# Turning the scaled keys of items 8 and up on VectorE instead of TensorE

## The chip, the cores and the metric

The kernel runs on one core of a Trainium2 chip. Its time is the device time of one execution in microseconds. It has five engines that work side by side: TensorE (PE: products, weights loaded by PEld), VectorE (DVE), ScalarE (ACT), GpSimd (POOL) and SyncE (SP, which only starts transfers here).

## The reference

Gated linear attention and two layers of a fully connected network behind it, all in float32. Batch 4, 8 heads, 768 positions, 48 numbers per head:

```python
f = 1.0 / (1.0 + np.exp(-f_logit))
for t in range(S):
    state = f[:, :, t, :, None] * state + np.einsum('bhd,bhe->bhde', k[:, :, t], v[:, :, t])
    y[:, :, t] = np.einsum('bhd,bhde->bhe', q[:, :, t], state)
# x = y as 3072 tokens x 384
h = x @ w_in                                   # 384 -> 2048
g = np.where(h >= 1, h, np.where(h <= -1, 0.0, (h + 1) ** 2 / 4))
x = g @ w_out                                  # 2048 -> 384
h = x @ w_in2
P = a[0] + a[1] * h + a[2] * h**2 + a[3] * h**3
Q = 1.0 + abs(b[0]) * abs(h) + abs(b[1]) * h**2
out = (P / (Q + 1e-06)) @ w_out2
```

## The kernel before

The attention is cut into 24 items: six chunks of 128 positions, each for four pairs of heads (GROUPS = 4; ITEMS = 24). An item holds two heads of all four batches. Keys, queries and gates lie with the head's 48 numbers on the partitions (one head at 0, the other at 64) and 4 x 128 positions as columns.

For each item the running product of the gates is formed (`scan`, L846, VectorE), the keys are multiplied by its inverse growth (`scale_keys`, L511, GpSimd, into k_s) and the queries divided by it (`newton`, `scale_queries`, L862 to L873, VectorE). TensorE then makes the scores inside the chunk (`scores`, L1066), VectorE masks them (`mask`, L885), and TensorE makes the outputs, from the state that the chunk starts with (L1080) and from the masked scores (L1085). The state is carried on by `deltas` (L1096): a product of keys and values over the 128 positions. For this the keys must have positions on the partitions, so k_s is turned: four 128x128 transposes on TensorE (`transposes`, L1050, into the PSUM bank at_bank) and a copy to SBUF by ScalarE (`copy_keys`, L614, into k_nat). VectorE adds the product to the state (`states`, L899). The last chunk needs no new state: items 20 to 23 have neither transposes nor state products.

The first network layer pair runs in 96 tiles of 128 hidden units x 512 tokens. A tile n is nine products into PSUM (`spline_first`, L1126), then ScalarE's ReLU and square (L646, L649), VectorE's join (`spline_join`, L917), ScalarE's rounding into a high part (L656), VectorE's rest (`spline_lo`, L925), and nine products into the accumulators (`spline_second`, L1143). TensorE runs the second products two tiles behind the first (LAG1 = 2). The second pair of layers follows with the lines L1165 and L1187.

From item 4 on each item is worked off inside a window of four tiles, item i = 4 + n // 4, at fixed stages n % 4. Nothing schedules the work but the order of the code on each engine, with semaphores between engines. TensorE runs in stage 0 the first products of the tile, the transposes and the scores of item i, and the second products of an older tile; in stage 1 only the products of tiles; in stage 2 first products, outputs and state products, then second products; in stage 3 products of tiles. VectorE runs in stage 0 the join, the mask of item i, the rest and the scan of item i + 1; in stage 1 the join and the rest; in stage 2 join, rest and the query scaling of item i + 1; in stage 3 the rest of y and the state addition of item i, then join and rest. k_s has two buffers, k_nat one: the copy into it waits until the state products of the item before have read it (delta_ready), and GpSimd scales the keys of item i + 2 only when item i has been turned (kt_ready) and its scores made.

Of the kernel before, what the change touches and what calls it, by code (L numbers as in the profile page):

```python
# [11 lines left out]
P = 128  # L12
BATCH, HEADS, SEQ, DH = 4, 8, 768, 48
HS = 64
PAIRS = BATCH * HEADS // 2
CK = 128
NC = SEQ // CK
# [33 lines left out]
GROUPS = 4  # L51
# [59 lines left out]
def build(nc, qT, kT, fT, vT, fC, kC, qC, vC, w1, w2, a, b, outT):  # L111
# [3 lines left out]
    with ctx:  # L115
# [171 lines left out]
        def k_natural(i):  # L287
            return k_nat_head if i == HEAD - 1 else k_nat

        def values(i):  # L290

            if 2 <= i < HEAD:
                return v_head[i - 2], v_loaded[i], 16, -1
            turn = i // 2 - (i >= HEAD)
            return v_in[i % 2], v_loaded[i % 2], 16 * (turn + 1), i - HEAD if i < HEAD + 2 else i - 2
# [190 lines left out]
        def _(pool):  # L486
# [14 lines left out]
            def scale_keys(i):  # L501
                if i >= ITEMS:
                    return
                u = i % 2
                pool.wait_ge(k_loaded[u], 32 * (i // 2 + 1))
                pool.wait_ge(growth_ready, GROUPS * (i + 1))
                before = i - HEAD if i < HEAD + 2 else i - 2
                if before >= 0:
                    pool.wait_ge(scores_ready, before + 1)
                    pool.wait_ge(kt_ready, min(before + 1, ITEMS - GROUPS))  # L510
                nc.gpsimd.tensor_tensor(k_scaled(i)[:, :], k_in[u][:, :], growth[u][:, :], ALU.mult).then_inc(k_ready, 1)  # L511

            def split_w1(k):
# [68 lines left out]
        def _(act):  # L582
# [24 lines left out]

            def copy_keys(i):
                if i >= ITEMS - GROUPS:
                    return  # L610
                if i > 0 and i != HEAD - 1:
                    act.wait_ge(delta_ready, i)
                act.wait_ge(kt_ready, i + 1)
                nc.scalar.copy(k_natural(i)[:, :], misc_at(i)).then_inc(knat_ready, 1)  # L614
# [208 lines left out]
        def _(dve):  # L823
# [10 lines left out]
            def scan(i):  # L834
                if i >= ITEMS:
                    return
                u = i % 2
                chunk, r = chunk_of(i)
                dve.wait_ge(step_ready, i + 1)
                if chunk > 0:  # L840
                    dve.wait_ge(ends_done, i - GROUPS + 1)
                for b in range(BATCH):
                    at = slice(b * CK, (b + 1) * CK)
                    col = BATCH * r + b
                    before = ends[:, col:col + 1] if chunk > 0 else 1.0
                    nc.vector.tensor_tensor_scan(growth[u][:, at], growth[u][:, at], zero[:, 0:1].to_broadcast([P, CK]),  # L846
                                                 before, ALU.mult, ALU.add).then_inc(growth_ready, 1)
                dve.wait_ge(growth_ready, GROUPS * (i + 1))
                last = growth[u][:, :].rearrange("p (b t) -> p b t", b=BATCH)[:, :, CK - 1:CK]
                nc.vector.tensor_copy(ends[:, BATCH * r:BATCH * (r + 1)].rearrange("p (b t) -> p b t", t=1),  # L850
                                      last).then_inc(ends_done, 1)
# [24 lines left out]
            def mask(i):  # L876
# [4 lines left out]
                for h in range(2):  # L881
# [2 lines left out]
                    tri = causal[:, :].rearrange("p (b t) -> p b t", b=1).to_broadcast([P, BATCH, CK])  # L884
                    nc.vector.tensor_tensor(dst, src, tri, ALU.mult).then_inc(masked, 1)  # L885

            def states(i):
                chunk, r = chunk_of(i)
                if i >= ITEMS - GROUPS:
                    return  # L890
                if i < GROUPS:
                    dve.wait_ge(state_set, r + 1)
                dve.wait_ge(delta_ready, i + 1)
                dve.wait_ge(y_done, i + 1)
                for h in range(2):
                    at = slice(HS * h, HS * h + DH)
                    term = misc_at(i)[at, 0:BATCH * DH].rearrange("p (b e) -> p b e", e=DH)
                    total = state[r][at, :, HS * h:HS * h + DH]
                    nc.vector.tensor_tensor(total, total, term, ALU.add).then_inc(delta_done, 1)  # L899
# [105 lines left out]
            for n in range(WINDOW, N1):  # L1005
                i, stage = window_of(n)
                if stage == 3:
                    rest_y(i)
                    states(i)
                spline_join(n)  # L1010
                if stage == 0:
                    mask(i)
                spline_lo(n)
                if stage == 0:
                    scan(i + 1)
                if stage == 2:
                    newton(i + 1)
                    scale_queries(i + 1)
                if n == TILES:
                    dve.wait_ge(coef_loaded, 32)  # L1020
                    nc.vector.scalar_tensor_tensor(out=b_abs[:, :], in0=b_bc[:, :], scalar=-1.0, in1=b_bc[:, :],
                                                   op0=ALU.mult, op1=ALU.max).then_inc(b_abs_set, 1)
                if n == N1 - TILES:
                    dve.wait_ge(ends_done, ITEMS)
                    nc.vector.tensor_scalar(ok[:, 0:PAIRS], ends[:, :], MAX_GROWTH, None, ALU.is_le).then_inc(ok_done, 1)
                    dve.wait_ge(ok_done, 1)
                    nc.vector.tensor_reduce(ok[:, PAIRS:PAIRS + 1], ok[:, 0:PAIRS], axis=AX.X, op=ALU.min).then_inc(ok_done, 1)
                if n == N1 - TILES + 4:
                    dve.wait_ge(ok_sum, 1)
                    nc.vector.tensor_copy(okflag[0:1, 0:1], at_bank[0:1, 0:1]).then_inc(flag_set, 1)  # L1030
# [7 lines left out]
        @block.tensor  # L1038
        def _(pe):
            def transposes(i):  # L1040
                if i >= ITEMS - GROUPS:
                    return
                pe.wait_ge(k_ready, i + 1)
                if i < HEAD:
                    pe.wait_ge(masked, 2 * (i + 1))
                elif i > HEAD:
                    pe.wait_ge(delta_done, 2 * i)
                for b in range(BATCH):
                    at = slice(b * CK, (b + 1) * CK)
                    mm = nc.tensor.transpose(misc_at(i)[:, at], k_scaled(i)[:, at], ident[:, :])  # L1050
                mm.then_inc(kt_ready, 1)
# [37 lines left out]
            def deltas(i):  # L1089
                if i >= ITEMS - GROUPS:  # L1090
                    return
                pe.wait_ge(knat_ready, i + 1)
                for b in range(BATCH):
                    for h in range(2):
                        keys = k_natural(i)[:, b * CK + HS * h:b * CK + HS * h + DH]
                        mm = nc.tensor.matmul(misc_at(i)[HS * h:HS * h + DH, b * DH:(b + 1) * DH], keys,  # L1096
                                              values(i)[0][:, b, h, :], start=True, stop=True)
                mm.then_inc(delta_ready, 1)
# [431 lines left out]
```

## Time and profile before

| | us |
|---|---|
| median of 3 runs | 920.63 (918.63 to 921.02) |
| profiled execution | 919.6 |
| its span | 917.9 |
| TensorE busy | 888.4 (97%) |
| VectorE busy | 663.6 (72%) |
| ScalarE busy | 632.2 (69%) |
| GpSimd busy | 276.8 (30%) |

Times of the profile are counted from the start of the span. An engine's busy time is the time in which it has an instruction under way; a matmul's own duration (about 390 ns for 512 columns) is longer than the distance from one to the next (0.23 us), since they overlap. The chain of waits counts each piece of time once: it follows the work that ended last back through whatever released it. The windows of items 8 to 19 lie between about 121 and 371 us, each some 20.6 us long.

### The profile page before, as it was taken

To read this page: it belongs to the slowest core of one execution; us is meant where nothing else is said; L and a number is where in the kernel's file an instruction comes from. 1 tells how busy PE (TensorE), PEld (TensorE's weight loads), DVE (VectorE), ACT (ScalarE), POOL (GpSimd) and SP (SyncE) were. 2 spreads that over 40 slices of the span, in tenths; PEclk is the share of its full clock that TensorE was granted. 3 is DMA by queue.
4 is the path that set the end of the run, shared out by engine and by line. 5 is a ranking of instruction groups with operands and counts; after the bars stand their busy time and mean duration, and the time that the engine had idled before them with its cause. 6 is when DMAs were issued, how large, how long until landed. Compare 5 with 4: busy or idle time off the path is not lost.

```text
span 917.9 us, 13209 instructions
## 1 busy us (share of the span) xinstructions
PE 888.4 (97%) x4786; PEld 733.2 (80%) x4786; DVE 663.6 (72%) x813; ACT 632.2 (69%) x821; POOL 276.8 (30%) x202
## 2 busy tenths in 40 slices
PE   4889999999999999999999999999999999999997
PEld 3668878888888888888887887888888888888885
DVE  8866666655655566555344799999889889899884
ACT  5656665566555655654577788888787887887872
POOL 4434510000010000000055385634344244353233
PEclk9989999999999999999999999999999999999999
DMA  7643113112211311110234121001001001000001
GB/s 208 170 115 120 44 35 103 46 35 64 58 35 36 86 50 52 59 40 1 69 104 126 50 66 35 1 35 35 0 34 34 23 11 34 34 0 0 34 0 39
DMA packets 27513, 48.72 MB, mean 53 GB/s; under 512 B 5312, under 2 KB 8384, under 8 KB 27456
## 3 DMA queue, kind: packets, MB, share of 16 engines
q1 hardware_dynamic: 27456, 48.00, 17.3%
q8 instruction: 31, 0.51, 0.2%
q14 instruction: 26, 0.21, 0.1%
HBM read 36.18 MB, written 9.44 MB: 50 GB/s over the span
## 4 chain that ended last, share of the span: by engine, by line
PE 82%; DVE 8%; ACT 4%; issue 4%; POOL 1%; POOLq 0%; DMA 0%; DVEq 0%; SPq 0%; ACTq 0%
PE acc L1143 19%; PE acc L1187 18%; PE h_pair L1126 18%; PE at_pair L1165 10%; PE h_pair L1165 10%; PE at_pair L1066 3%; PE at_pair L1085 2%; DVE growth L846 2%; PE at_pair L1080 2%; DVE g L917 1%; POOL g_lo L546 1%; PE at_bank L1050 1%; DVE probs L885 1%; ACT t L649 1%; ACT t L646 1%
## 5 line engine op out<-in xcount | busy, mean ns | idle before, releaser
L546 POOL TENSOR_TENSOR g_lo<-g,g_hi 128x1024 fp32r<-128x1024 f32 x48 | 116.8, 2434 | 217.1 <-DVE t L946 212.6
L917 DVE SCALAR_TENSOR_TENSOR g<-h_pair,t 128x512 f32<-128x512 f32 x96 | 66.4, 691 | 140.7 <-ACT t L649 140.5
L646 ACT ACTIVATE t<-h_pair,half 128x512 f32<-128x512 f32 x96 | 66.0, 688 | 104.8 <-PE h_pair L1126 103.6
L1126 PE MATMUL h_pair<-x_hi,w_hi 128*128 128x512 f32 x288 | 113.0, 392 | 3.1 <-DVE x_lo L910 2.3
L511 POOL TENSOR_TENSOR k_s<-k_in,growth 128x512 f32<-128x512 f32 x22 | 29.0, 1318 | 287.3 <-DVE growth L846 271.3
L1187 PE MATMUL acc<-g_hi,w_hi 128*128 128x512 f32 x288 | 112.4, 390 | 1.8 <-POOL g_lo L546 1.8
L1126 PE MATMUL h_pair<-x_hi,w_lo 128*128 128x512 f32 x288 | 112.2, 389 | 0.0
L1126 PE MATMUL h_pair<-x_lo,w_hi 128*128 128x512 f32 x288 | 112.1, 389 | 0.0
L1187 PE MATMUL acc<-g_lo,w_hi 128*128 128x512 f32 x288 | 112.1, 389 | 0.0
L1187 PE MATMUL acc<-g_hi,w_lo 128*128 128x512 f32 x288 | 112.0, 389 | 0.0
L1143 PE MATMUL acc<-g_hi,w_hi 128*128 128x512 f32 x264 | 108.0, 409 | 0.0
L656 ACT CAST g_hi<-g 128x512 fp32r<-128x512 f32 x88 | 54.6, 621 | 74.8 <-DVE g L917 74.8
L1143 PE MATMUL acc<-g_hi,w_lo 128*128 128x512 f32 x264 | 103.5, 392 | 0.0
L1143 PE MATMUL acc<-g_lo,w_hi 128*128 128x512 f32 x264 | 103.3, 391 | 0.0
L925 DVE TENSOR_TENSOR g_lo<-g,g_hi 128x512 fp32r<-128x512 f32 x88 | 62.9, 715 | 45.3 <-ACT g_hi L656 45.3
L937 DVE SCALAR_TENSOR_TENSOR s<-s,b_abs,g 128x1024 f32<-128x1024 f32 x48 | 69.4, 1445 | 31.9 <-ACT g L702 31.8
L525 POOL TENSOR_TENSOR w_lo<-w_raw,w_hi 128x256 fp32r<-128x256 f32 x48 | 48.2, 1031 | 69.8 <-ACT w_hi L640 66.3
L1126 PEld LDWEIGHTS h_pair<-x_hi,w_hi 128*128 128x128 f32 x288 | 54.0, 188 | 15.7 <-DVE x_lo L910 2.9
L1187 PEld LDWEIGHTS acc<-g_hi,w_hi 128*128 128x128 f32 x288 | 54.1, 188 | 14.2 <-POOL g_lo L546 3.1
L961 DVE SCALAR_TENSOR_TENSOR g<-g,a_bc,t 128x1024 f32<-128x1024 f32 x48 | 63.6, 1325 | 0.0
L1126 PEld LDWEIGHTS h_pair<-x_hi,w_lo 128*128 128x128 f32 x288 | 54.1, 188 | 11.4
L1187 PEld LDWEIGHTS acc<-g_hi,w_lo 128*128 128x128 f32 x288 | 54.1, 188 | 11.4
(142 smaller groups left out, 2038.7 us busy)
## 6 DMA issues: line engine op xcount, KB each, us to landing
w_raw<-w SPq DMA_DIRECT2D x32, 384.0 KB, 3.9
f_in<-fC SPq DMA_DIRECT2D x48, 96.0 KB, 2.8
k_in<-kC SPq DMA_DIRECT2D x48, 96.0 KB, 2.5
q_in<-qC SPq DMA_DIRECT2D x48, 96.0 KB, 2.2
mlp_out<-o_sb SPq DMA_DIRECT2D x18, 256.0 KB, 2.9
x_raw<-mlp_out SPq DMA_DIRECT2D x6, 768.0 KB, 4.5
outT<-o_sb SPq DMA_DIRECT2D x18, 256.0 KB, 2.0
v_in<-vC SPq DMA_DIRECT2D x22, 192.0 KB, 2.5
```

What stands on the lines that cost most here:

```text
L525: nc.gpsimd.tensor_tensor(w_lo[:, at], w_raw[:, at], w_hi[:, at].bitcast(F32), ALU.subtract).then_inc(w2_lo_done, 1)
L546: nc.gpsimd.tensor_tensor(g2_lo[r][:, :, :], g2[r][:, :, :], g2_hi[r][:, :, :].bitcast(F32), ALU.subtract).then_inc(lo2_ready, 1)
L646: nc.scalar.activation(t1[n % 2][:, :], h1[n % 2], ACT.Relu, scale=0.5, bias=half[:, :]).then_inc(relu1_ready, 1)
L656: nc.scalar.copy(hi, g1[n % 2][:, :]).then_inc(hi1_ready, 1)
L917: nc.vector.scalar_tensor_tensor(out=g1[n % 2][:, :], in0=h1[n % 2], scalar=1.0, in1=t1[n % 2][:, :], op0=ALU.max, op1=ALU.min).then_inc(g ...
L925: nc.vector.tensor_tensor(lo, g1[n % 2][:, :], hi.bitcast(F32), ALU.subtract).then_inc(lo1_ready, 1)
L937: nc.vector.scalar_tensor_tensor(out=s, in0=s, scalar=b_abs[:, 1:2], in1=g, op0=ALU.mult, op1=ALU.add).then_inc(den_ready, 1)
L961: nc.vector.scalar_tensor_tensor(out=g_before, in0=g_before, scalar=a_bc[:, 0:1], in1=t_before, op0=ALU.add, op1=ALU.mult).then_inc(g2_rea ...
L1126: mm = nc.tensor.matmul(h1[n % 2], w[:, at:at + P], x[:, kt, cols], start=(kt == 0 and j == 0), stop=(kt == KT - 1 and j == 2))
L1143: mm = nc.tensor.matmul(acc[o][:, :], w[:, at:at + P], g, start=(t == 0 and j == 0), stop=(t == TILES - 1 and j == 2))
L1165: mm = nc.tensor.matmul(h2[m % 2][:, c * NB:(c + 1) * NB], w[:, at:at + P], x[:, kt, xcols], start=(k == 0), stop=(k == 3 * KT - 1))
L1187: mm = nc.tensor.matmul(acc[o][:, :], w[:, at:at + P], g[m % R2][:, c, :], start=(m == 0 and c == 0 and k == 0), stop=(last and c == UW - ...
```

## The change

The turning of items 8 and up goes from TensorE and ScalarE to VectorE. `turned(i)` is true for i >= 2 * GROUPS = 8; with the last four items having none, these are the twelve items 8 to 19. `turn_keys(i)` stands in VectorE's stage 1, behind that tile's rest (L925). It runs 16 instructions, one for each 32 x 32 block position: q counts the 32 partitions of k_s that are read, j the 32 positions that become partitions of k_nat, and each instruction does this for the four batches (32 partitions, 4 x 32 columns). It reads k_s and writes k_nat, both in SBUF. The state products now wait for the sixteenth, and, as the transposes did, for the state addition of the item before.

```diff
@@ -12,6 +12,7 @@
 P = 128
 BATCH, HEADS, SEQ, DH = 4, 8, 768, 48
 HS = 64
+SQ = 32
 PAIRS = BATCH * HEADS // 2
 CK = 128
 NC = SEQ // CK
@@ -287,6 +288,10 @@
         def k_natural(i):
             return k_nat_head if i == HEAD - 1 else k_nat
 
+        def turned(i):
+
+            return i >= 2 * GROUPS
+
         def values(i):
 
             if 2 <= i < HEAD:
@@ -507,7 +512,10 @@
                 before = i - HEAD if i < HEAD + 2 else i - 2
                 if before >= 0:
                     pool.wait_ge(scores_ready, before + 1)
-                    pool.wait_ge(kt_ready, min(before + 1, ITEMS - GROUPS))
+                    if turned(before):
+                        pool.wait_ge(knat_ready, min(before + 1, ITEMS - GROUPS))
+                    else:
+                        pool.wait_ge(kt_ready, before + 1)
                 nc.gpsimd.tensor_tensor(k_scaled(i)[:, :], k_in[u][:, :], growth[u][:, :], ALU.mult).then_inc(k_ready, 1)
 
             def split_w1(k):
@@ -607,6 +615,8 @@
 
             def copy_keys(i):
                 if i >= ITEMS - GROUPS:
+                    return
+                if turned(i):
                     return
                 if i > 0 and i != HEAD - 1:
                     act.wait_ge(delta_ready, i)
@@ -884,6 +894,18 @@
                     tri = causal[:, :].rearrange("p (b t) -> p b t", b=1).to_broadcast([P, BATCH, CK])
                     nc.vector.tensor_tensor(dst, src, tri, ALU.mult).then_inc(masked, 1)
 
+            def turn_keys(i):
+                if i >= ITEMS - GROUPS or not turned(i):
+                    return
+                dve.wait_ge(k_ready, i + 1)
+                dve.wait_ge(delta_ready, i)
+                for q in range(P // SQ):
+                    src = k_scaled(i)[q * SQ:(q + 1) * SQ, :].rearrange("p (b t) -> p b t", b=BATCH)
+                    for j in range(CK // SQ):
+                        dst = k_natural(i)[j * SQ:(j + 1) * SQ, :].rearrange("p (b t) -> p b t", b=BATCH)
+                        mm = nc.vector.transpose(dst[:, :, q * SQ:(q + 1) * SQ], src[:, :, j * SQ:(j + 1) * SQ])
+                mm.then_inc(knat_ready, 1)
+
             def states(i):
                 chunk, r = chunk_of(i)
                 if i >= ITEMS - GROUPS:
@@ -1013,6 +1035,8 @@
                 spline_lo(n)
                 if stage == 0:
                     scan(i + 1)
+                if stage == 1:
+                    turn_keys(i)
                 if stage == 2:
                     newton(i + 1)
                     scale_queries(i + 1)
@@ -1038,7 +1062,7 @@
         @block.tensor
         def _(pe):
             def transposes(i):
-                if i >= ITEMS - GROUPS:
+                if i >= ITEMS - GROUPS or turned(i):
                     return
                 pe.wait_ge(k_ready, i + 1)
                 if i < HEAD:
@@ -1090,6 +1114,8 @@
                 if i >= ITEMS - GROUPS:
                     return
                 pe.wait_ge(knat_ready, i + 1)
+                if turned(i):
+                    pe.wait_ge(delta_done, 2 * i)
                 for b in range(BATCH):
                     for h in range(2):
                         keys = k_natural(i)[:, b * CK + HS * h:b * CK + HS * h + DH]
```

VectorE around stages 1 and 2 of item 14's window, before (k_s_91 is k_s of even items, g_lo the second part of a tile, growth and guess belong to item 15):

```order
L917 SCALAR_TENSOR_TENSOR g_1_98<-h_pair,t_1_96 128x512 [waits lo1_ready,s1_ready]
L925 TENSOR_TENSOR g_lo_104<-g_1_98,g_hi_101 128x512 [waits multiplied1,hi1_ready]
L917 SCALAR_TENSOR_TENSOR g_0_97<-h_pair,t_0_95 128x512 [waits lo1_ready,s1_ready]
L925 TENSOR_TENSOR g_lo_102<-g_0_97,g_hi_99 128x512 [waits multiplied1,hi1_ready]
L862 TENSOR_TENSOR q_s_90<-growth_86,guess_88 128x512 [waits y_done,guess_ready]
L864 SCALAR_TENSOR_TENSOR guess_88<-q_s_90,guess_88 128x512 [waits newton_done]
L873 SCALAR_TENSOR_TENSOR q_s_90<-guess_88,q_in_82 128x512 [waits q_loaded1,inv_ready]
L910 TENSOR_TENSOR x_lo<-at_pair,x_hi 48x512 [waits yhi_done]
```

And now, where L939, L947, L872, L874, L883 and L932 are the old L917, L925, L862, L864, L873 and L910:

```order
L939 SCALAR_TENSOR_TENSOR g_1_98<-h_pair,t_1_96 128x512 [waits lo1_ready,s1_ready]
L947 TENSOR_TENSOR g_lo_104<-g_1_98,g_hi_101 128x512 [waits multiplied1,hi1_ready]
L906 STREAM_TRANSPOSE k_nat<-k_s_91 32x4x32 [waits delta_ready,k_ready]
L906 STREAM_TRANSPOSE k_nat<-k_s_91 32x4x32 x15
L939 SCALAR_TENSOR_TENSOR g_0_97<-h_pair,t_0_95 128x512 [waits lo1_ready,s1_ready]
L947 TENSOR_TENSOR g_lo_102<-g_0_97,g_hi_99 128x512 [waits multiplied1,hi1_ready]
L872 TENSOR_TENSOR q_s_90<-growth_86,guess_88 128x512 [waits y_done,guess_ready]
L874 SCALAR_TENSOR_TENSOR guess_88<-q_s_90,guess_88 128x512 [waits newton_done]
L883 SCALAR_TENSOR_TENSOR q_s_90<-guess_88,q_in_82 128x512 [waits q_loaded1,inv_ready]
L932 TENSOR_TENSOR x_lo<-at_pair,x_hi 48x512 [waits yhi_done]
```

Sixteen transposes stand between the rest of the window's second tile and the join of its third; the order of all else is the same.

TensorE in stage 0 of the same window, from the last first-layer product to the second-layer products, before:

```order
L1126 MATMUL h_pair<-x_hi,w_lo 128x512
L1050 MATMUL at_bank<-ident,k_s_91 128x128 [waits delta_done,k_ready]
L1050 MATMUL at_bank<-ident,k_s_91 128x128 x3
L1066 MATMUL at_pair<-q_s_89,k_s_91 128x128 [waits ylo_done,q_ready,k_ready]
L1066 MATMUL at_pair<-q_s_89,k_s_91 128x128 x7
L1143 MATMUL acc<-g_hi_101,w_hi 128x512 [waits lo1_ready]
```

And now (L1152 is the old L1126, L1090 the old L1066, L1169 the old L1143):

```order
L1152 MATMUL h_pair<-x_hi,w_lo 128x512
L1090 MATMUL at_pair<-q_s_89,k_s_91 128x128 [waits ylo_done,q_ready,k_ready]
L1090 MATMUL at_pair<-q_s_89,k_s_91 128x128 x7
L1169 MATMUL acc<-g_hi_101,w_hi 128x512 [waits lo1_ready]
```

The four transposes are gone, and the scores follow the tile directly.

TensorE in stage 2, from the outputs to the second-layer products, before:

```order
L1080 MATMUL at_pair<-q_s_89,state_74 128x128 [waits delta_done,v_loaded0,masked]
L1080 MATMUL at_pair<-q_s_89,state_74 128x128 x3
L1085 MATMUL at_pair<-probs_93,v_in_83 48x128 x8
L1096 MATMUL at_bank<-v_in_83,k_nat 48x48 [waits knat_ready]
L1096 MATMUL at_bank<-v_in_83,k_nat 48x48 x7
L1143 MATMUL acc<-g_hi_100,w_hi 128x512 [waits lo1_ready]
```

And now (L1104, L1109 and L1122 are the old L1080, L1085 and L1096):

```order
L1104 MATMUL at_pair<-q_s_89,state_74 128x128 [waits delta_done,v_loaded0,masked]
L1104 MATMUL at_pair<-q_s_89,state_74 128x128 x3
L1109 MATMUL at_pair<-probs_93,v_in_83 48x128 x8
L1122 MATMUL at_bank<-v_in_83,k_nat 48x48 [waits delta_done,knat_ready]
L1122 MATMUL at_bank<-v_in_83,k_nat 48x48 x7
L1169 MATMUL acc<-g_hi_100,w_hi 128x512 [waits lo1_ready]
```

No instruction moved here; the state products have one more wait.

## Rows read from the trace of the kernel before

**Rows 1.** The page, busy time of each engine

```profile
PE 888.4 (97%) x4786; PEld 733.2 (80%) x4786; DVE 663.6 (72%) x813; ACT 632.2 (69%) x821; POOL 276.8 (30%) x202
```

**Rows 2.** Busy time by stage, 175 to 450 us: stretch, length, PE, PEld, DVE, ACT, POOL, clock

```profile
175.00:450.00 275.00, 275.00 (x1712) 228.42 (x1711) 158.11 (x278) 155.28 (x254) 15.46 (x12) 1.00 0.17 49
```

**Rows 3.** The chain of waits: start us, length us, engine, tile, line

```profile
247.12 0.44 PE at_bank L1050 x4
247.55 1.09 PE at_pair L1066 x16
248.64 2.28 PE acc L1143 x9
...
258.95 0.36 PE at_bank L1096 x16
...
267.70 0.44 PE at_bank L1050 x4
...
370.63 1.09 PE at_pair L1066 x16
...
390.40 1.09 PE at_pair L1066 x16
```

**Rows 4.** Timeline of VectorE, item 14's window: start us, length us, operation

```profile
249.14 1.28 DVE L885 TENSOR_TENSOR probs<-at_pair,causal 128x512 f32<-128x512 f32 x2
...
255.77 0.69 DVE L925 TENSOR_TENSOR g_lo<-g,g_hi 128x512 fp32r<-128x512 f32 x1 [0.69 <-ACT g_hi L656]
258.47 0.69 DVE L917 SCALAR_TENSOR_TENSOR g<-h_pair,t 128x512 f32<-128x512 f32 x1 [2.00 <-ACT t L649]
259.85 0.69 DVE L925 TENSOR_TENSOR g_lo<-g,g_hi 128x512 fp32r<-128x512 f32 x1 [0.69 <-ACT g_hi L656]
260.46 0.69 DVE L862 TENSOR_TENSOR q_s<-growth,guess 128x512 f32<-128x512 f32 x1
...
263.94 0.74 DVE L899 TENSOR_TENSOR state<-state,at_bank 48x192 f32<-48x192 f32 x2
```

**Rows 5.** Groups of instructions by shape: busy us, mean ns, idle before

```profile
L846 DVE TENSOR_TENSOR_SCAN growth<-growth,ends,zero 128x128 f32<-128x128 f32 x80 | 36.2, 514 | 0.0
...
L885 DVE TENSOR_TENSOR probs<-at_pair,causal 128x512 f32<-128x512 f32 x42 | 26.9, 682 | 3.6 <-PE at_pair L1066 3.6
...
L899 DVE TENSOR_TENSOR state<-state,at_bank 48x192 f32<-48x192 f32 x32 | 11.2, 351 | 0.9
...
L614 ACT COPY k_nat<-at_bank 128x512 f32<-128x512 f32 x16 | 9.1, 569 | 0.0
...
L850 DVE COPY ends<-growth 128x4 f32<-128x4 f32 x24 | 4.1, 170 | 0.8
```

**Rows 6.** Timeline of TensorE, the state products of item 14

```profile
258.78 0.53 PE L1096 MATMUL at_bank<-v_in,k_nat 128*48 128x48 f32 x16
```

**Rows 7.** The chain of waits around 56 us

```profile
56.37 0.14 issue
56.51 1.09 PE at_bank L1050 x4
57.59 2.01 PE at_pair L1066 x16
59.61 3.41 PE acc L1143 x9
```

**Rows 8.** Timeline of TensorE, two stops; in brackets idle time before

```profile
56.51 1.09 PE L1050 MATMUL at_bank<-ident,k_s 128*128 128x128 f32 x4 [3.52 <-DVE state L899]
...
121.25 0.50 PE L1126 MATMUL h_pair<-x_hi,w_hi 128*128 128x512 f32 x1 [2.00 <-DVE x_lo L910]
```

**Rows 9.** Busy time and granted clock by stage around those stops

```profile
53.00:55.20 2.20, 0.00 (x0) 0.00 (x0) 1.03 (x3) 1.31 (x3) 1.52 (x2) 1.00 0.00 0
55.20:62.00 6.80, 5.49 (x26) 4.49 (x27) 4.79 (x9) 4.71 (x8) 3.76 (x5) 0.50 0.17 36
115.00:125.00 10.00, 8.00 (x48) 6.27 (x46) 7.41 (x11) 5.32 (x10) 2.27 (x3) 1.00 0.19 52
```

## The prediction

> **What bounds the kernel now.** I read the page's busy line first: TensorE is busy in 97% of the span, VectorE in 72% [rows 1]. The stage table says it more sharply: from 175 to 450 us TensorE is busy for 275.00 of 275 us at a granted clock of 1.00, VectorE for 158.11 [rows 2]. Then the chain of waits through one item's window (item 14, 247.12 to 267.70 us): its steps are TensorE's, one behind the other; the group shows those that count here [rows 3]. So in the changed stretch a microsecond off TensorE is a microsecond off the end, and VectorE has room on average. What has to be asked is whether it has room at the one place where its result is wanted.
>
> The diff's condition is i >= 8, bounded only by the 20 items that have keys to turn. It therefore changes items 8 to 19, twelve windows, not the eight that "items 8 to 15" suggests. All numbers below are for twelve.
>
> **What goes.** Four transposes of 128x128 per item take 0.44 us of the chain [rows 3]. Item 20 has neither transposes nor state products, and its window confirms it: from one group of scores to the next it takes 390.40 - 370.63 = 19.77 us, against 267.70 - 247.12 = 20.58 for item 14 with both; the difference, 0.81, is 0.44 of transposes and 0.36 of state products [rows 3]. Twelve items: 12 x 0.44 = 5.3 us off TensorE. ScalarE's copy (569 ns) goes too; it lies beside TensorE's work, no step of ScalarE is in the chain there, and I cost it at nothing [rows 2, 5]: ScalarE is busy for 155.28 of the 275 us. The order table shows only the transposes gone from TensorE's queue: the state products keep their place, right behind the outputs, in front of the second-layer products of the tile.
>
> **What comes, and its price.** VectorE gets 16 transposes per item, each of 32 partitions x 128 elements, 192 in all. The trace has none, so I bound one from rows. Two-input operations of 512 and 192 elements take 682 and 351 ns [rows 5]: (682 - 351) / 320 = 1.03 ns an element, so 128 elements make 351 - 66 = 285 ns. How far apart they start depends on whether they overlap. The two masks, one behind the other, both starting at partition 0, take 1.28 us together, so the second starts 1.28 - 0.68 = 0.60 us after the first, before that one's 0.68 is over. The two state additions start at partitions 0 and 64; they take 0.74 together, so the second starts 0.74 - 0.35 = 0.39 after the first, 0.04 behind its end [rows 4, 5]. The transposes change their target partitions with each instruction, so I take them as the second kind: 0.285 + 0.04 = 0.325, rounded up to 0.33 us, 16 x 0.33 = 5.3 us per item. As the first kind: 0.60 - 384 x 1.03 ns = 0.20 us, 3.2 us per item. Still lower is the shortest such instruction of the trace, 0.17 us with 4 elements (2.7 us per item) [rows 5]; below that I see no reason. The upper end is the scan, which spends 514 ns on 128 elements, as a transpose of 4-byte data could: 0.55 with the gap, 8.8 us per item [rows 5].
>
> The Trainium skill bears on this twice. "VectorE: DVE Perf Modes", section "Two Vector instructions with no wait between them", has a rule: an instruction whose input or output starts in another group of 32 partitions than that of the one before starts only when all earlier ones have finished. By this rule 15 of the 16 are held and the item costs 16 x 0.325 = 5.2 us; without it 3.2. The trace agrees: 0.39 for the state pair of which the masks' 0.60 would make about 0.27. The same page, "The three transpose paths", gives 311 ns for VectorE's blocks and 390 ns for TensorE's 128x128, which reads as if VectorE were the cheaper place. An estimate from that page for our 16 pieces, with the gap of 0.04, is 5.6 us, because its figure is for one instruction on 128 partitions and this code uses 32 at a time; TensorE's 0.44 for four [rows 3] is far below four times its 390 ns. By that 5.6 the sum below would be 12 x 0.3 = 3.6 us higher.
>
> **Where the price falls due.** The transposes stand on VectorE behind the rounding (L925) of the window's second tile. In item 14's window L925 starts at 255.77, and the operation behind such an L925 starts 0.61 us later (259.85, then 260.46) [rows 4]. So they would start at 256.38. What they release, the state products, start on TensorE at 258.78, the outputs in front of them ending at 258.95 in the chain [rows 3, 6]. From the end of a VectorE operation to the released matmul the trace has 0.14 us (the issue piece from 56.37 to 56.51 [rows 7]). With 5.3 us the products start at 256.38 + 5.3 + 0.14 = 261.82: a shift of 3.04 us, of which 261.82 - 258.95 = 2.87 is a stop of TensorE. The room is 258.78 - 256.38 = 2.40 us, so with d for the distance between transposes the break-even is 16 d + 0.14 - 2.40 = 0.44, d = 0.17 us.
>
> Is this paid again by others? Queued behind the transposes are the join of the third tile (L917, 258.47), then its rounding, the next item's scaling, x_lo and the state addition, which starts at 263.94 and takes 0.74 [rows 4]. They shift by 256.38 + 5.3 - 258.47 = 3.2 us, so x_lo is there by 267.2 and VectorE free at 267.9. TensorE has stood still as well and arrives at the next scores, which want q_s and x_lo, at 267.70 + 3.0 = 270.7 at the earliest. The fourth tile's join follows the first layer on TensorE, which is later by those 3.0 us, too. So one stall per window, no second one. GpSimd's scaling of the next keys waits for the transposes of the item before, done a window earlier: nothing. The second of the two waits in front of the state products (state addition of the item before) was there already, in front of the transposes that go. In the window the distance from the first layer's end to L925 to the state products is set by TensorE and ScalarE, and it is the same in items 8 to 19.
>
> Sum: 12 x (3.04 - 0.44) = 31.2 us. Against the profiled execution, 919.6 us for a span of 917.9, that is 950.8.
>
> **TensorE's clock.** A stop of TensorE has a price of its own here. Before 56.51 us it stood still for 3.52 us; some 2.2 us into the stop the granted clock fell from 1.00 to 0.50 (2.4 to 1.2 GHz) and was still there up to 62 us [rows 8, 9]. The work after the stop took 1.09 + 2.01 + 3.41 us where the same three groups take 0.44 + 1.09 + 2.28 [rows 3, 7]: 2.70 us lost. The stop of 2.00 us in front of 121.25 left the clock at 1.00 [rows 8, 9]. The new stops, 2.87 us, lie between. If none has it the time is 951; if all twelve, 12 x 2.70 = 32 more, 983. The two rows do not say more than that it is in between; I take four of twelve, 11 us: 962 for the profiled execution, 963 against the median of 920.6, which is 1.0 above the profiled 919.6.
>
> **The rivals.** (a) The stall is as computed and the clock holds: 951 to 952. For it: the 2.00 us stop. Against: the clock fell 2.2 us into the longer one. (b) The transposes overlap, 0.20 each: shift 3.2 + 0.14 - 2.40 = 0.94, net 0.50 x 12 = 6 us, stops under 1 us, so no clock price: 926 to 927. For it the mask pair, against it the state pair. (c) Faster: VectorE's 2.4 us of room before the state products holds the transposes, d below 0.17; then the whole 5.3 us of TensorE are won: 915. For it: VectorE is idle for 2.00 us before the third tile's join, just behind the place of the transposes [rows 4]. Against: no such operation of the trace is shorter than 0.17. It decides at 16 d = 2.7 us. (d) Four-byte transposes at the scan's pace, 0.55: shift 8.8 + 0.14 - 2.40 = 6.5, net 6.1 x 12 = 73, with every stop long enough for the clock, 32: 1025. (e) Items 8 to 15 only, contrary to the code: two thirds of the price, 948.
>
> **How the numbers follow.** Forecast (stall, clock falls in some windows) 0.54; (a) 0.25; (b) 0.08; (c) 0.03; (d) 0.08; (e) 0.02. The forecast's own range, d from 0.30 to 0.36 with two to twelve falls: 0.30 gives 4.8 and a net of 2.1 x 12 = 25 + 5, 950; 0.36 gives 5.8 and 3.1 x 12 = 37 + 32, 989. The range takes in (a) and (e), and leaves (b), (c) and (d) out, 0.19 together: 940 to 990. A measurement of this kernel tells about 0.3% (2.8 us) from no change; (c) alone is faster, 0.03, with 0.02 for a d right at the break-even, and 0.95 slower.
>
> **What would show it.** Right: 192 transposes of about 0.29 us, starting 0.33 apart; the state products waiting for them, twelve waits of 2.9 us; window 23.2 us instead of 20.6; granted clock 0.50 behind some of the stops; nothing new in front of the scores. Wrong: transposes starting 0.20 or 0.55 apart, twelve windows shorter than 20.6, a second wait per window in front of the scores or of the first layer, or clocks all at 1.00.

## The result, and the profile after

| | before | after |
|---|---|---|
| median | 920.59 us (4 runs) | 970.06 us (4 runs, 968.12 to 971.07) |
| ratio | 1 | 1.0542, 95% interval 1.0528 to 1.0556 |
| profiled execution, span | 919.6, 917.9 | 971.07, 969.0 |
| TensorE busy | 888.4 (97%) | 908.7 (94%) |
| VectorE busy | 663.6 | 720.4 |

The kernel became 5.4% slower: 49.5 us, where 42 had been forecast (962, range 940 to 990). From the page of the changed kernel: busy time, the slices of VectorE, the granted clock in tenths in 40 slices, and the chain of waits by engine.

```profile
PE 908.7 (94%) x4738; PEld 744.4 (77%) x4738; DVE 720.4 (74%) x1005; ACT 626.9 (65%) x809; POOL 277.3 (29%) x202
...
DVE  8856677666666666656533479999989989889884
...
PEclk9989998999899999999999999999999999999999
...
PE 71%; DVE 14%; ACT 7%; issue 6%; POOL 1%; POOLq 0%; DMA 0%; DVEq 0%; SPq 0%; ACTq 0%
```

Slices 6 to 17 of VectorE, with the twelve items, now stand at 6 and 7 tenths. Slices 7 and 11 of the clock show an 8, where all from the fourth on showed a 9 before. Of the chain 14% are VectorE's; before it was 8%.

What a transpose costs, from the groups by shape (busy us, mean ns, idle before), and where the block stands in item 14's window, from VectorE's timeline (start us, length us):

```profile
L906 DVE STREAM_TRANSPOSE k_nat<-k_s 32x128 f32<-32x128 f32 x192 | 58.0, 302 | 2.4
```

```profile
282.20 0.69 DVE L947 TENSOR_TENSOR g_lo<-g,g_hi 128x512 fp32r<-128x512 f32 x1 [0.69 <-ACT g_hi L666]
282.81 5.04 DVE L906 STREAM_TRANSPOSE k_nat<-k_s 32x128 f32<-32x128 f32 x16
287.88 0.69 DVE L939 SCALAR_TENSOR_TENSOR g<-h_pair,t 128x512 f32<-128x512 f32 x1
```

192 transposes, as the order of the instructions says, so items 8 to 19. One takes 302 ns and sixteen take 5.04 us: (5.04 - 0.30) / 15 = 0.316 us from one to the next. The block starts 0.61 us behind the rest L947, and the third tile's join starts when it ends. The same place in the chain of waits (start us, length us):

```profile
279.44 0.70 ACT t L656
...
280.16 0.64 ACT t L659
...
280.82 0.70 DVE g L939
...
281.55 0.63 ACT g_hi L666
...
287.54 0.32 DVE k_nat L906
...
287.90 0.56 PE at_bank L1122 x16
288.47 3.72 PE acc L1169 x9
```

The same products in the kernel before:

```profile
259.31 2.27 PE acc L1143 x9
```

In [rows 3] this stretch was TensorE's alone. Now it goes from a first-layer tile through ScalarE (L656, L659), VectorE's join, ScalarE's rounding and sixteen transposes, and comes back to TensorE at 287.90. There the state products start 0.05 us behind the last transpose. The second-layer products behind them take 3.72 us instead of 2.27: a lower clock. From TensorE's waits (us in total, times, longest), then the windows of items 13, 14 and 20 from one group of scores to the next (stretch, length, PE, PEld, DVE, ACT, POOL, clock, DMA), the answer to [rows 3]:

```profile
PE at_bank L1122 <- DVE k_nat L906: 30.3, 12, 2.5
```

```profile
248.26:274.00 25.74, 23.22 (x131) 18.80 (x130) 17.06 (x38) 11.25 (x18) 1.29 (x1) 0.87 0.19 53
274.00:298.46 24.46, 21.94 (x130) 17.81 (x130) 17.06 (x38) 11.25 (x18) 1.29 (x1) 0.93 0.12 33
...
421.86:441.63 19.77, 19.77 (x114) 16.20 (x114) 10.91 (x19) 12.03 (x20) 1.29 (x1) 1.00 0.20 66
```

Twelve stops of 2.52 us. The windows of items 8 to 19 take 24.3 to 24.5 us, and three of them 25.7, where all took about 20.6; each has a mean clock of 0.93 or 0.87. Item 20's is 19.77 as in [rows 3], and from its scores to the end of the span it is 547.1 us, against 547.3 (from 370.63) before: behind the twelve windows nothing changed its pace. In front of them this execution is 1.0 us late (in the chain item 8's scores start at 125.01 instead of 124.03), which is no more than executions of the kernel before differ by (918.63 to 921.02).

### The profile page after: what moved, and what is told of

It is laid out like the page before. It is cut to its first block, busy times and chain, and to the rows that moved or that the text cites. A ratio compares the mean times of both kernels' runs of the same rounds, so it can differ in the third digit from the quotient of the medians.

```text
span 969.0 us, 13293 instructions
## 1 busy us (share of the span) xinstructions
PE 908.7 (94%) x4738; PEld 744.4 (77%) x4738; DVE 720.4 (74%) x1005; ACT 626.9 (65%) x809; POOL 277.3 (29%) x202
## 4 chain that ended last, share of the span: by engine, by line
PE 71%; DVE 14%; ACT 7%; issue 6%; POOL 1%; POOLq 0%; DMA 0%; DVEq 0%; SPq 0%; ACTq 0%
PE acc L1169 17%; PE acc L1213 17%; PE h_pair L1152 14%; PE at_pair L1191 9%; PE h_pair L1191 9%; DVE k_nat L906 5%; PE at_pair L1090 2%; DVE g L939 2%; ACT t L656 2%; DVE growth L856 2%; ACT t L659 2%; ACT g_hi L666 1%; PE at_bank L1122 1%; POOL g_lo L554 1%; DVE guess L874 1%
## 5 line engine op out<-in xcount | busy, mean ns | idle before, releaser
L939 DVE SCALAR_TENSOR_TENSOR g<-h_pair,t 128x512 f32<-128x512 f32 x96 | 66.4, 692 | 131.4 <-ACT t L659 130.9
L656 ACT ACTIVATE t<-h_pair,half 128x512 f32<-128x512 f32 x96 | 66.1, 688 | 123.3 <-PE h_pair L1152 120.9
L1152 PE MATMUL h_pair<-x_hi,w_hi 128*128 128x512 f32 x288 | 114.5, 398 | 3.2 <-DVE x_lo L932 2.5
L1169 PE MATMUL acc<-g_hi,w_hi 128*128 128x512 f32 x264 | 115.5, 438 | 0.0
L1213 PE MATMUL acc<-g_hi,w_hi 128*128 128x512 f32 x288 | 112.4, 390 | 1.9 <-POOL g_lo L554 1.9
L1152 PE MATMUL h_pair<-x_hi,w_lo 128*128 128x512 f32 x288 | 112.9, 392 | 0.0
L1152 PE MATMUL h_pair<-x_lo,w_hi 128*128 128x512 f32 x288 | 112.9, 392 | 0.0
L1213 PE MATMUL acc<-g_lo,w_hi 128*128 128x512 f32 x288 | 112.1, 389 | 0.0
L1213 PE MATMUL acc<-g_hi,w_lo 128*128 128x512 f32 x288 | 112.1, 389 | 0.0
L1169 PE MATMUL acc<-g_lo,w_hi 128*128 128x512 f32 x264 | 110.4, 418 | 0.0
L1169 PE MATMUL acc<-g_hi,w_lo 128*128 128x512 f32 x264 | 110.2, 418 | 0.0
L947 DVE TENSOR_TENSOR g_lo<-g,g_hi 128x512 fp32r<-128x512 f32 x88 | 62.9, 715 | 45.3 <-ACT g_hi L666 45.3
L1152 PEld LDWEIGHTS h_pair<-x_hi,w_hi 128*128 128x128 f32 x288 | 55.3, 192 | 16.5 <-DVE x_lo L932 3.0
L1169 PEld LDWEIGHTS acc<-g_hi,w_hi 128*128 128x128 f32 x264 | 54.1, 205 | 14.6 <-issue 1.0
L1213 PEld LDWEIGHTS acc<-g_hi,w_hi 128*128 128x128 f32 x288 | 54.0, 188 | 14.3 <-POOL g_lo L554 3.1
L1152 PEld LDWEIGHTS h_pair<-x_lo,w_hi 128*128 128x128 f32 x288 | 55.2, 192 | 11.6
```

The costliest lines, as they stand in the source:

```text
L656: nc.scalar.activation(t1[n % 2][:, :], h1[n % 2], ACT.Relu, scale=0.5, bias=half[:, :]).then_inc(relu1_ready, 1)
L939: nc.vector.scalar_tensor_tensor(out=g1[n % 2][:, :], in0=h1[n % 2], scalar=1.0, in1=t1[n % 2][:, :], op0=ALU.max, op1=ALU.min).then_inc(g ...
L947: nc.vector.tensor_tensor(lo, g1[n % 2][:, :], hi.bitcast(F32), ALU.subtract).then_inc(lo1_ready, 1)
L1152: mm = nc.tensor.matmul(h1[n % 2], w[:, at:at + P], x[:, kt, cols], start=(kt == 0 and j == 0), stop=(kt == KT - 1 and j == 2))
L1169: mm = nc.tensor.matmul(acc[o][:, :], w[:, at:at + P], g, start=(t == 0 and j == 0), stop=(t == TILES - 1 and j == 2))
L1213: mm = nc.tensor.matmul(acc[o][:, :], w[:, at:at + P], g[m % R2][:, c, :], start=(m == 0 and c == 0 and k == 0), stop=(last and c == UW - ...
```

## The experiments

Two things were open. First, how the 49.5 us divide between the stall of the state products and the lower clock behind it; the prediction had the clock fall in four windows, and the trace shows it in twelve. Second, whether the place of the block makes it dear (theory A) or the work of 60 us added to VectorE (theory B). Beside these stood the question of what sets the 0.316 us. The kernels with fewer transposes leave out part of the turning, and the one whose transposes keep to their partitions writes the turned keys to other places than the products read; these three have one execution each.

**TensorE kept busy through the stop.** In `deltas`, in front of the wait for the turned keys:

```diff
-                pe.wait_ge(knat_ready, i + 1)
                 if turned(i):
                     pe.wait_ge(delta_done, 2 * i)
+                    cols = x_cols((i - HEAD) * WINDOW // TILES)
+                    for r in range(10):
+                        nc.tensor.matmul(at_bank[:, :], w_hi[:, 0:P], x_hi[:, 0, cols], start=True, stop=True)
+                pe.wait_ge(knat_ready, i + 1)
```

> The changed kernel, but in front of the wait for the turned keys TensorE runs ten products of 512 columns (2.3 us) into the PSUM bank that the state products overwrite afterwards, in items 8 to 19. The state products start when the transposes end, as in the changed kernel; only the stop is filled. If the clock price is that of the stop itself: clock 1.00, windows 22.9 us, 947 us. If the remaining 20 us have another cause (the later first layer, the joins): still 965 to 970 us.

Measured: 948.49 us, ratio 1.0307 (1.0292 to 1.0323). Stage table from 120 to 420 us, and two scores in the chain, items 14 and 15:

```profile
120.00:420.00 300.00, 297.70 (x1793) 239.97 (x1793) 217.56 (x481) 151.70 (x247) 16.77 (x13) 1.00 0.17 50
```

```profile
262.03 1.09 PE at_pair L1090 x16
...
284.93 1.09 PE at_pair L1090 x16
```

The window is 22.90 us and the clock 1.00, as expected. Useless work makes the kernel 21.6 us faster than the changed one, by the medians. So the stall is worth 948.49 - 919.64 = 28.9 us (919.64 is the median of the kernel before, 15 runs taken together with this one) and the clock 970.06 - 948.49 = 21.6 us. The traces give nearly the same: from item 8's scores to item 20's it is 246.6 us before, 274.8 with the stop filled, 296.9 in the changed kernel, so 28.2 and 22.1.

**Shorter stops.** Fourteen and twelve of the sixteen transposes; for twelve:

```diff
                 for q in range(P // SQ):
+                    if q >= 3:
+                        continue
```

> As the changed kernel, but the last two of the sixteen transposes of each item are left out: block 4.4 us, stop of TensorE 1.89 us. If the clock holds: net 1.66 us per window, 919.6 + 20 = 940 us. If it falls behind every stop: 963 us. In between, some windows have it and some not.

> As the changed kernel, but the last four of the sixteen transposes of each item (the last 32 partitions of the keys) are left out, so VectorE's block is 12 x 0.316 = 3.8 us and TensorE's stop 1.26 us instead of 2.52. If the clock holds through a stop of this length: net 1.03 us per window, 919.6 + 12.3 = 932 us, clock 1.00. If it falls behind every stop, whatever its length: 1.9 us more per window, 955 us.

Measured, one run each: 960.13 us with fourteen, 932.69 us with twelve. Waits of TensorE and clocks, first with fourteen (windows of items 14 and 15, the ten others take 23.81 to 23.85 us, all at 0.93), then with twelve (one stretch over the windows of items 8 to 19, 258.85 / 12 = 21.57 us each):

```profile
PE at_bank L1124 <- DVE k_nat L908: 22.6, 12, 1.9
```

```profile
268.17:291.99 23.82, 21.94 (x130) 17.78 (x130) 16.44 (x36) 11.25 (x18) 1.29 (x1) 0.93 0.12 34
291.99:315.84 23.85, 21.97 (x130) 17.81 (x130) 16.44 (x36) 11.25 (x18) 1.29 (x1) 0.93 0.12 34
```

```profile
PE at_bank L1124 <- DVE k_nat L908: 15.0, 12, 1.3
```

```profile
124.91:383.76 258.85, 243.86 (x1539) 199.80 (x1538) 188.28 (x407) 138.04 (x224) 15.50 (x12) 1.00 0.18 51
```

With twelve stops of 1.88 us the clock fell in all twelve windows; with twelve stops of 1.25 us in none. The 932.69 is what the stall alone was to give, the 960.13 lies 3 us under the figure with the clock falling each time: its windows lose 23.83 - 21.57 - 2 x 0.316 = 1.6 us to the clock, not 1.9.

**Transposes that keep to their partitions.**

```diff
-                        dst = k_natural(i)[j * SQ:(j + 1) * SQ, :]...
-                        mm = nc.vector.transpose(dst[:, :, q * SQ:(q + 1) * SQ], src[...])
+                        dst = k_natural(i)[q * SQ:(q + 1) * SQ, :]...
+                        mm = nc.vector.transpose(dst[:, :, j * SQ:(j + 1) * SQ], src[...])
```

> As the changed kernel, with sixteen transposes of the same shape, but each group of four reads and writes the same 32 partitions (the turned keys land in other places than the products want). If an instruction is held only because its input or output starts in another group of 32 partitions than the one before: 12 of 16 overlap and start 0.20 us apart, block 12 x 0.20 + 4 x 0.316 = 3.7 us, stop 1.1 us, 931 us with the clock holding. If transposes never overlap each other: still 0.316 apart, 5.04 us, and 970 us as the changed kernel.

Measured, one run: 930.02 us. VectorE's timeline, the block of item 14:

```profile
260.90 3.57 DVE L906 STREAM_TRANSPOSE k_nat<-k_s 32x128 f32<-32x128 f32 x16
```

3.57 us instead of 5.04 for the same sixteen shapes. If the three changes of partitions keep 0.316, the twelve other steps take (3.57 - 0.30 - 0.95) / 12 = 0.19 us. The distance of 0.316 was the price of changing the 32 partitions with each instruction. By the Trainium skill's rule on held instructions ("VectorE: DVE Perf Modes", section "Two Vector instructions with no wait between them") the same follows, and the two runs agree with it: 0.32 us held, 0.19 not held.

**The block in another place.** All sixteen, but for item i + 1 in stage 3 of the window before, a window's half earlier than wanted:

```diff
-                if stage == 1:
-                    turn_keys(i)
+                if stage == 3:
+                    turn_keys(i + 1)
```

> The sixteen VectorE transposes of item i+1 stand in stage 3 of item i's window, behind the rest of that window's last tile, instead of in stage 1 of the item's own window; nothing else differs from the changed kernel. Theory A (the price is the place: the state products wait 2.5 us per window for them, and the clock falls behind each stop): the transposes are done some 14 us before they are wanted, no stop of TensorE in the windows of items 8 to 19, clock 1.00 there, windows 20.15 us, and the 12 x 0.44 us of TensorE are won: 915 us, ratio to the kernel before 0.994. Theory B (60 us more work on VectorE slow the tiles wherever it stands, through the join or the rest of a tile that TensorE wants): new waits of TensorE for g or g_lo, 1 us or more per window, 927 us or more.

Measured: 933.30 us, ratio 1.0149 (1.0135 to 1.0164). No state product waits any more, and the clock falls only twice (near 294 and 379 us) instead of twelve times, yet it is slower than before, so theory A is wrong as it stood. TensorE's waits from 120 to 400 us, VectorE's timeline around the block, and the chain of waits behind an earlier one:

```profile
PE h_pair L1152 <- DVE x_lo L932: 7.5, 4, 2.0
PE h_pair L1152 <- DVE g L939: 4.2, 6, 0.9
```

```profile
188.03 0.69 DVE L947 TENSOR_TENSOR g_lo<-g,g_hi 128x512 fp32r<-128x512 f32 x1 [0.69 <-ACT g_hi L666]
188.64 5.04 DVE L906 STREAM_TRANSPOSE k_nat<-k_s 32x128 f32<-32x128 f32 x16
193.72 0.69 DVE L939 SCALAR_TENSOR_TENSOR g<-h_pair,t 128x512 f32<-128x512 f32 x1
```

```profile
178.44 0.61 issue
179.05 0.68 ACT t L656
179.75 0.64 ACT t L659
180.41 0.70 DVE g L939
181.14 0.63 ACT g_hi L666
```

The chain hardly touches TensorE. The join of a window's first tile comes only when the block is done (172.39, and 193.72 one window on), masks and scan follow it, and the second tile's join comes at 176.50. ScalarE works in the order of its code: behind that join it makes the rounding, then the next item's guess (L611, 177.76), and only at 179.05 the third tile's ReLU and square, though TensorE had finished that tile at 175.5. So each tile's join waits for the one before, through ScalarE's queue, and this window takes 21.3 us (from the join at 172.39 to that at 193.72), above the 20.15 of a TensorE that never waits. The twelve windows take 20.1 to 25.0 us, 21.6 in the mean. The longest, those of items 11, 15 and 19, are the ones in which the first-layer products stop for x_lo, 1.81 to 1.85 us, and in two of these three the clock falls behind the stop. VectorE was not full, busy for 201.9 of the 259.4 us of the twelve windows: what hurt was 5 us in one piece.

**The same with items 6 and 7 too** (turned from i >= 6):

> As the run with the transposes in stage 3 of the window before, but for items 6 to 19, fourteen instead of twelve. Theory A: another 2 x 0.44 us off TensorE, 914 us. Theory B: the windows of items 6 and 7 are those in which the chain of waits of the kernel before goes through VectorE (scan, masks, query scaling), so 5 us more in each come in full: 920 to 925 us.

Measured: 935.71 us, ratio 1.0177 (1.0164 to 1.0191), 2.4 us more than from item 8 on. My two cases both started from a base that had already failed. Around items 6 to 8 TensorE stops twice for x_lo, 2.31 us in front of 102.57 and 4.23 us in front of 126.53, and the clock falls behind both.

**The products moved instead of the block.** TensorE in stage 2:

```diff
                 if stage == 2:
-                    second_half(i)
+                    outputs(i)
+                    if not turned(i):
+                        deltas(i)
                 if n not in HOLD:
                     spline_second(due)
                     due += 1
+                if stage == 2 and turned(i):
+                    deltas(i)
```

> The transposes stay in stage 1 on VectorE as in the changed kernel, but TensorE runs the state products of items 8 to 19 behind the second-layer products of stage 2 instead of in front of them, so 2.27 us later. Theory A: the stop shrinks from 2.52 to about 0.25 us and the clock stays at 1.00; 919.6 - 5.3 + 12 x 0.4 = 919 us. Theory B: VectorE's block of 5 us in stage 1 holds up the third tile's join as before, and that costs by itself: 927 us or more, with waits of TensorE for g.

Measured: 927.10 us, ratio 1.0082 (1.0069 to 1.0095). The stops shrank as expected, and the clock was 1.00 from 120 to 400 us:

```profile
PE at_bank L1122 <- DVE k_nat L906: 5.5, 12, 0.7
```

These 5.5 us, less the 5.3 of the transposes, leave the time where it was. Where the other 7 us are shows against the kernel further down in which TensorE never waits. Its twelve windows take 241.5 us, all of them busy; here they take 255.1 with 247.7 busy:

```profile
122.73:377.83 255.10, 247.74 (x1538) 198.63 (x1537) 201.95 (x455) 135.26 (x223) 15.55 (x12) 1.00 0.18 52
```

So TensorE stands still for 7.4 us (the 5.5, and 0.61 us for x_lo in each of three windows) and its own work takes 6.2 us more. The chain of waits here, too, runs on from the transposes through join, rounding, scaling and ScalarE's queue, so in both moves the block of 5 us stands in the chain. How much of the 6.2 us is the block's and how much comes with the new order of the products no run separates.

**The block dealt out into VectorE's idle time.** Here `turn_keys(i, first, last)` runs instructions first to last - 1 of the sixteen; the waits stand in front of the first of them, the release behind the sixteenth.

```diff
                 if stage == 0:
                     mask(i)
+                if stage == 3:
+                    turn_keys(i + 1, 0, 2)
+                if stage == 1:
+                    turn_keys(i, 10, 12)
                 spline_lo(n)
+                if stage == 3:
+                    turn_keys(i + 1, 2, 6)
                 if stage == 0:
                     scan(i + 1)
+                    turn_keys(i, 6, 10)
                 if stage == 1:
-                    turn_keys(i)
+                    turn_keys(i, 12, 16)
```

> The sixteen transposes of an item are dealt out to places where VectorE idles in the kernel before: 2 between the join and the rest of the stage-3 tile of the window before (it waits 0.69 us there for ScalarE's rounding), 4 behind that rest (2.01 us idle), 4 behind the scan of stage 0 (1.65), 2 between join and rest of stage 1 (0.69), 4 behind that rest (2.00, of which 2.4 lie before the state products). Each piece takes 0.316 us times its number, so 0.63 and 1.26 us. If what made the run with all sixteen in stage 3 slow (933 us) is one block of 5 us in a row of steps between VectorE and ScalarE: TensorE never waits in the windows of items 8 to 19, the clock holds, 919.6 - 5.3 = 914 to 916 us. If it is VectorE's load as a sum: again over 925 us.

Measured: 914.58 us, ratio to the kernel before 0.9949 (0.9936 to 0.9963). VectorE's timeline in stages 0 and 1 of a window, and the stage table from 175 to 450 us, the answer to [rows 2]:

```profile
230.23 1.25 DVE L907 STREAM_TRANSPOSE k_nat<-k_s 32x128 f32<-32x128 f32 x4
231.49 0.69 DVE L941 SCALAR_TENSOR_TENSOR g<-h_pair,t 128x512 f32<-128x512 f32 x1
232.21 0.62 DVE L907 STREAM_TRANSPOSE k_nat<-k_s 32x128 f32<-32x128 f32 x2
232.87 0.69 DVE L949 TENSOR_TENSOR g_lo<-g,g_hi 128x512 fp32r<-128x512 f32 x1
233.60 1.26 DVE L907 STREAM_TRANSPOSE k_nat<-k_s 32x128 f32<-32x128 f32 x4
```

```profile
175.00:450.00 275.00, 275.00 (x1689) 227.34 (x1684) 202.48 (x426) 152.72 (x248) 15.52 (x12) 1.00 0.17 49
```

VectorE's busy time in that stretch rises from 158.11 to 202.48 us, TensorE's stays at 275.00 of 275, the clock at 1.00, and the whole 5.3 us of TensorE's transposes are gained (919.64 - 914.58 = 5.1). The two transposes between join and rest take the time in which VectorE waited for ScalarE's rounding. Theory B is out: the same load, in pieces of 0.6 and 1.3 us, costs nothing.

**The spread from item 6 on.**

> The same spread, for items 6 to 19. If the windows of items 6 and 7 have idle time in the same places: 0.9 us less than the spread from item 8 on. They are the ones whose chain of waits runs over VectorE before, so I expect up to 5 us more instead: 915 to 920 us.

Measured: 918.93 us, ratio 0.9988 (0.9979 to 0.9997), 4.4 us more than from item 8. TensorE waits for the turned keys twice:

```profile
PE at_bank L1131 <- DVE k_nat L907: 5.1, 2, 3.0
```

The clock falls behind the longer of the two stops: it is 0.50 from 118 to 121 us. VectorE has idle time in the window of item 6 as a sum (it was busy for 14.3 of 20.9 us), but none behind the scan, where four transposes were put. From VectorE's timeline of the kernel before:

```profile
85.39 2.96 DVE L846 TENSOR_TENSOR_SCAN growth<-growth,ends,zero 128x128 f32<-128x128 f32 x4
...
88.46 0.69 DVE L917 SCALAR_TENSOR_TENSOR g<-h_pair,t 128x512 f32<-128x512 f32 x1
```

The scan takes 2.96 us here, where it takes 1.6 in the later windows, and the second tile's join follows at once. Why it is slower here was not tested.

## Why the prediction was right, and where a term was off

- What bounds it: right. Item 20's window kept its 19.77 us, and with TensorE never waiting (the spread) 5.1 of its 5.3 us came off the end.
- Twelve items, not eight: right, by 192 transposes.
- Price of a transpose: 0.33 us forecast, 0.316 measured; 5.3 us a block against 5.04. The reason given, that instructions which change their partitions do not overlap, was shown by the run that keeps them (3.57 us).
- The stall: the shift of the state products was put at 3.04 us. Measured from the rest of the second tile: 258.78 - 255.77 = 3.01 us before [rows 4, 6], 287.90 - 282.20 = 5.70 after, a shift of 2.69. Of the 0.35 too much, 0.26 are the block (5.3 against 5.04), 0.09 the release, 0.05 us instead of 0.14. The sum of 31.2 us for stall and gain stands against 28.9 measured with the clock held.
- Paid once per window: right. TensorE had no second wait in a window; with the stop filled the window was 22.90 us, which is 20.58 + 2.32, where 2.60 had been forecast.
- TensorE's clock: the term that was mis-sized. "I take four of twelve, 11 us": it fell in twelve of twelve and cost 21.6 us, 1.8 each rather than 2.70. The number taken for four was a guess between two rows, a stop of 3.52 us that had a fall and one of 2.00 that had none. In this place 1.88 us were enough. The 2.70 us, too, came from a single fall: three windows lost 2.8 us, the nine others 1.5. That the forecast came so near is in part luck, for the two errors work against each other: twelve falls at 2.70 would have been 32 us, and 983.
- Rivals: (a), the clock holding, forecast 951 to 952, is the kernel with the stop filled, 948.49. (b), transposes that overlap, forecast 926 to 927, is near the run that keeps the partitions, 930.02. (d) is out: one transpose takes 302 ns and they start 0.316 us apart, not 0.55. (e) is out, by 192 transposes. (c), VectorE's room holding the transposes, was false for one block of 5 us, and its figure of 915 came true when they were spread over more room than the prediction had looked at.
- Range: 970 lies inside. It is above the 962 because the clock cost 10.6 us more than the 11 put down for it; the stall cost 2.3 us less.

What stays open is why the stop of 2.00 us at 121.25 [rows 8] left the clock alone while every one of 1.88 us did not. The runs do show that between 1.8 and 2.0 us the length of the stop does not decide it alone. In the run with the block in stage 3 the same products stop at the same place in three windows, for 1.81, 1.84 and 1.85 us; behind the first the clock holds, behind the two others it falls. The first two, and the clock around them:

```profile
207.24 0.50 PE L1152 MATMUL h_pair<-x_hi,w_hi 128*128 128x512 f32 x1 [1.81 <-DVE x_lo L932]
293.18 0.50 PE L1152 MATMUL h_pair<-x_hi,w_hi 128*128 128x512 f32 x1 [1.84 <-DVE x_lo L932]
```

```profile
205.40:212.00 6.60, 4.79 (x32) 3.77 (x32) 5.71 (x14) 3.14 (x6) 0.00 (x0) 1.00 0.10 31
294.50:297.00 2.50, 2.50 (x9) 1.56 (x10) 1.77 (x6) 2.13 (x4) 0.00 (x0) 0.50 0.00 0
```

From item 6 on, two stops there of 1.85 us differ as well: a fall behind the one in front of 212.55, none behind the one in front of 298.49. Of all stops between 60 and 430 us in these traces, none of up to 1.25 us had a fall and all of 2.3 us and more had one. No run varied the work in front of a stop.

## What to carry to other kernels

Where one engine is the bound and another has over a quarter of its time free, the question is not whether the work fits into the sum but into which gap, and in pieces of what length: here the same sixteen instructions cost 49 us in one place, 14 in another, and gained 5 when dealt out. A stall of the bounding TensorE should be costed twice, once for its length and once for the clock behind it. And an engine that works its queue in order passes a delay on to jobs that do not depend on it; look behind the late instruction on each engine that waits for it.

## What the runs showed of the hardware that was not expected

The granted clock can fall after the work has resumed. In item 10's window TensorE stopped for 2.52 us and went on at 188.95; the stage table of the changed kernel shows the clock still high then:

```profile
189.00:190.00 1.00, 1.00 (x18) 0.87 (x19) 0.62 (x1) 0.35 (x1) 0.00 (x0) 0.97 0.00 0
190.00:193.00 3.00, 3.00 (x8) 2.34 (x7) 2.63 (x5) 1.33 (x3) 0.00 (x0) 0.50 0.43 115
...
194.00:199.00 5.00, 5.00 (x24) 4.12 (x23) 2.46 (x5) 2.72 (x5) 0.00 (x0) 1.00 0.16 48
```

It was 0.50 soon after 189.9, a microsecond into the work, and full again before 194. Six of the twelve falls came after the work had resumed, the six others in the last 0.6 us of the stop. With fourteen transposes all twelve came after it, the last of them 1.6 us into the work, which went on at 400.57:

```profile
400.57:402.00 1.43, 1.43 (x20) 1.24 (x21) 0.74 (x2) 0.73 (x2) 0.00 (x0) 1.00 0.04 11
402.50:405.00 2.50, 2.50 (x7) 1.96 (x6) 2.43 (x5) 0.48 (x1) 0.00 (x0) 0.50 0.61 184
```

So the clock column of a stage table has to be read beyond the end of the stop. The falls cost unequal amounts, too: nine windows of 24.3 to 24.5 us and three of 25.7 against 22.90 with the stop filled, so 1.5 or 2.8 us each. And a 32 x 128 transpose of float32 on VectorE costs less than a scan of as many elements, 302 against 514 ns [rows 5], in line with an ordinary operation of that size.
